# A three-stage kernel (WKV scan, MLP, routed experts) on one core: first expert's identity products, split order and one first level rearranged

## What is computed

```python
for t in range(S):                       # attention: B=2, H=8, S=768, D=48
    y[:, :, t] = r[t] . (state + (u*k[t]) outer v[t])
    state = w[t] * state + k[t] outer v[t]
x = relu(y @ w_in) ** 2 @ w_out          # MLP: 384 -> 2048 -> 384
expert = argmax(x @ w_gate)              # 8 experts, capacity 384 tokens each
out[i] = gate[i] * (relu(x[i] @ w1[expert]) @ w2[expert])   # 384 -> 1024 -> 384
```

## Time and profile before

| | |
|---|---|
| median of 3 runs | 496.4 us (495.31 to 496.63) |
| the profiled execution | 497.71 us |
| its span (first to last instruction) | 496.0 us |
| mean granted TensorE clock | 0.975 of full speed |
| TensorE busy | 457.9 us (92%) |
| VectorE busy | 317.0 us (64%) |
| ScalarE busy | 212.4 us (43%) |
| GpSimd busy | 53.6 us (11%) |

### The profile page before, as it was taken

How to read it: one execution, slowest core, us unless ns; L and a number is a source line. 1 busy time by engine, 2 the same in 40 slices (tenths; PEclk the granted TensorE clock), 3 DMA queues, 4 the chain that set the end, 5 groups by cost and what they waited for, 6 DMA issues and landing times.

```text
span 496.0 us, 15154 instructions
## 1 busy us (share of the span) xinstructions
PE 457.9 (92%) x6363; PEld 433.3 (87%) x6363; DVE 317.0 (64%) x805; ACT 212.4 (43%) x429; POOL 53.6 (11%) x64
## 2 busy tenths in 40 slices
PE   3678999999999999999999999998899988999993
PEld 3568989999999999999999899988899778989993
DVE  4985986777577756775677644435563778687510
ACT  2342463243523342434243444353365876676320
POOL 5000000000100010001000100101002334232301
PEclk9985999999999999999999999998899999999998
DMA  8941585680050005000000149201928798620000
GB/s 268 340 146 50 200 281 184 216 307 3 35 177 3 3 35 177 2 3 35 3 3 1 35 156 354 81 1 59 313 64 284 216 370 278 218 59 7 29 14 27
DMA packets 35356, 62.45 MB, mean 126 GB/s; under 512 B 3564, under 2 KB 21918, under 8 KB 35280
## 3 DMA queue, kind: packets, MB, share of 16 engines
q1 hardware_dynamic: 32976, 56.89, 33.9%
q0 software_dynamic: 2304, 4.47, 2.4%
HBM read 49.78 MB, written 14.19 MB: 129 GB/s over the span
## 4 chain that ended last, share of the span: by engine, by line
PE 70%; DVE 15%; issue 7%; ACT 4%; DMA 1%; SPq 0%; DVEq 0%; POOL 0%; ACTq 0%; POOLq 0%
PE bank L635 18%; PE bank L621 16%; PE bank L809 5%; PE pair L546 4%; PE pair L503 4%; PE bank L762 3%; PE pair L777 3%; PE bank L816 3%; PE bank L777 2%; DVE W L1021 2%; DVE KRW L1050 2%; DVE AD L1062 2%; PE pair L762 2%; DVE KRW L1049 2%; PE pair L567 2%
## 5 line engine op out<-in xcount | busy, mean ns | idle before, releaser
L621 PE MATMUL bank<-XH,W 128*128 128x256 f32 x576 | 121.9, 288 | 0.0
L635 PE MATMUL bank<-W,GH 128*128 128x384 f32 x384 | 102.3, 347 | 0.7 <-ACT X L848 0.7
L621 PEld LDWEIGHTS bank<-XH,W 128*128 128x128 f32 x576 | 96.3, 191 | 1.5 <-ACT RB L927 0.8
L848 ACT ACTIVATE GH<-GG 128x256 fp32r<-128x256 f32 x96 | 40.2, 419 | 115.6 <-DVE GG L1106 114.9
L621 PE MATMUL bank<-XL,W 128*128 128x256 f32 x288 | 81.5, 283 | 0.0
L1110 DVE TENSOR_TENSOR GL<-GG,GH 128x256 fp32r<-128x256 f32 x96 | 40.6, 423 | 41.9 <-ACT GH L848 41.9
L635 PEld LDWEIGHTS bank<-W,GH 128*128 128x128 f32 x384 | 64.1, 188 | 2.1 <-DVE GL L1110 1.0
L635 PE MATMUL bank<-W,GL 128*128 128x384 f32 x192 | 64.7, 337 | 0.0
L546 PE MATMUL pair<-KRW 48*64 48x32 f32 (+1 forms) x2304 | 48.1, 231 | 15.6 <-DMA KRW<-in_krw 6.4
L546 PEld LDWEIGHTS pair<-KRW 48*64 48x64 f32 (+1 forms) x2304 | 42.3, 146 | 22.9 <-issue 11.5
L927 ACT ACTIVATE RB<-bank 128x256 f32<-128x256 f32 x96 | 36.4, 379 | 44.4 <-PE bank L621 44.0
(11 more groups left out here) (139 smaller groups left out, 718.7 us busy)
## 6 DMA issues: line engine op xcount, KB each, us to landing
raw<-in_moe_w SPq DMA_DIRECT2D x23, 768.0 KB, 7.8
stage<-in_moe_w SPq DMA_DIRECT2D x9, 768.0 KB, 7.3
KRW<-in_krw SPq DMA_DIRECT2D x12, 512.0 KB, 6.1
slots<-X SPq DMA_DIRECT2D x8, 579.0 KB, 4.8
VV<-in_v SPq DMA_DIRECT2D x12, 288.0 KB, 9.2
XG<-slots SPq DMA_DIRECT2D x16, 193.0 KB, 3.1
KRW<-in_krw SPq DMA_DIRECT2D x12, 256.0 KB, 6.3
stage<-in_moe_w_in SPq DMA_DIRECT2D x4, 768.0 KB, 6.7
```

What stands on the lines that cost most here:

```text
L621: last = nc.tensor.matmul(bank[4 + f % 2][:, 0:2 * P], win[wa][:, c, f * P:(f + 1) * P], xa[:, c, :], start=n == 0, stop=n == 3 * KM - 1)
L635: last = nc.tensor.matmul(bank[6 + m][:, 0:DM], ga[f % G4][:, cols], wout[wa][:, f, :], start=f == 0 and n == 0, stop=f == NF - 1 and n == 2)
L848: return nc.scalar.activation(dst, src, ACT.Copy)
```

## The change

The slots of the first low splits become 5, 6, 7. On TensorE, level 0 and diagonal of group 1's tile 1 go behind `hidden(0, 0)`. The first expert's rows get banks `XB0` = 2, 3, 4; the identity products of tiles 0 and 1 are issued right behind the logits of the last group, ahead of its ranks; that of tile 2 stays where it was, and the wait for `rank_used` is gone. ScalarE and VectorE take all three tiles of expert 0's rows before the splits of chunks 2 and 3. VectorE's `gates` of expert 0 go behind its last `hidden_low` (or ahead of `hidden_low_small`, if that runs alone). The split of the last chunk of experts 4, 6 and 7 goes from behind f = 2 to behind f = 4, on both engines.

```diff
@@ -41,7 +41,7 @@
     KEYS = (10, 13)
     ZS, ZO = 8, 4
     HIGH_SLOT = (0, 1, 2, 3, 17, 19, 21, 23)
-    LOW_SLOT = (6, 7, 8, 18, 20, 22, 26, 29)
+    LOW_SLOT = (5, 6, 7, 18, 20, 22, 26, 29)
     ROWS, LOGITS, CHOOSE, RANKS, PLACE = range(5)
     GATE_SLOT = (4, 6, 7, 8, 9)
     PL = 3
@@ -135,6 +135,7 @@
         SB = (5, 2)
         SMALL = {0: (2, 4), 2: (7, 3)}
         XB = (0, 1, 4)
+        XB0 = (2, 3, 4)
         pair = [ctx.enter_context(nc.psum_tensor(f"pair{t}", [P, 2, 512], F32)) for t in range(2)]
         bank = [pair[n // 2][:, n % 2, :] for n in range(4)]
         bank += [ctx.enter_context(nc.psum_tensor(f"bank{n}", [P, 512], F32)) for n in range(4, 8)]
@@ -661,12 +662,18 @@
                                         start=False, stop=True)
                 last.then_inc(rank_done, 1)
 
+            def first_rows_early(m):
+
+                for q in range(KM):
+                    nc.tensor.matmul(bank[XB0[m]][:, q * P:(q + 1) * P], early[m][:, q * P:(q + 1) * P], ident[:, :],
+                                     start=q == 0, stop=False, skip_group_check=True)
+
             def attention(i, s, late):
 
                 n, k = due(i, s)
                 if n is None or late != (k == 0 or k > NL + 1):
                     return
-                for t in range(2):
+                for t in range(1 if (n, k) == (1, 0) else 2):
                     if k < NL:
                         level(n, t, k)
                     if k == 0:
@@ -684,6 +691,9 @@
                 for s in range(NF):
                     if mlp:
                         hidden(i - 1, s)
+                    if (i, s) == (1, 0):
+                        level(1, 1, 0)
+                        diagonal(1, 1)
                     if attn:
                         attention(i, s, False)
                     if mlp:
@@ -701,6 +711,11 @@
                         if attn:
                             pe.wait_ge(sel[0], NMASK * i + 4)
                         logits(i - 2)
+                        if i == NG + 1:
+                            pe.wait_ge(ld_early, 16 * MT)
+                            pe.wait_ge(relu_ready, NF * NG)
+                            for m in range(2):
+                                first_rows_early(m)
                     if RANKS in parts:
                         if attn:
                             pe.wait_ge(sel[0], NMASK * i + 5)
@@ -719,26 +734,16 @@
                 need(pe, xl2_ready, MT * e)
                 transposes(bank[XB[m]], XG[m], KM, xt2_done)
 
-            def first_rows_early(m):
-
-                for q in range(KM):
-                    nc.tensor.matmul(bank[XB[m]][:, q * P:(q + 1) * P], early[m][:, q * P:(q + 1) * P], ident[:, :],
-                                     start=q == 0, stop=False, skip_group_check=True)
-
             def first_rows_late(m):
 
                 for q in range(KM):
                     for n in range(2):
-                        last = nc.tensor.matmul(bank[XB[m]][:, q * P:(q + 1) * P], X2[:, n, q * P:(q + 1) * P],
+                        last = nc.tensor.matmul(bank[XB0[m]][:, q * P:(q + 1) * P], X2[:, n, q * P:(q + 1) * P],
                                                 chosen[n][:, m * P:(m + 1) * P], start=False, stop=n == 1,
                                                 skip_group_check=True)
                 last.then_inc(xt2_done, 1)
 
-            pe.wait_ge(ld_early, 16 * MT)
-            pe.wait_ge(rank_used, NG)
-            pe.wait_ge(relu_ready, NF * NG)
-            for m in range(MT):
-                first_rows_early(m)
+            first_rows_early(2)
             pe.wait_ge(slot_ready, NG)
             nc.tensor.matmul(bank[6][:, 0:NE], ones[:, :], earlier[:, 0, :], start=True, stop=True).then_inc(count_done, 1)
             pe.wait_ge(chosen_ready, 1)
@@ -944,12 +949,11 @@
             def rows_high(e, m):
                 act.wait_ge(xt2_done, MT * e + m + 1)
                 copy(XH2[:, :, m * P:(m + 1) * P],
-                     bank[XB[m]][:, 0:DM].rearrange("p (c n) -> p c n", c=KM)).then_inc(xh2_ready, 1)
-
-            for m in range(2):
+                     bank[(XB if e else XB0)[m]][:, 0:DM].rearrange("p (c n) -> p c n", c=KM)).then_inc(xh2_ready, 1)
+
+            for m in range(MT):
                 rows_high(0, m)
             split_high_expert(0, 2)
-            rows_high(0, 2)
             split_high_expert(0, 3)
 
             def hidden_high(e):
@@ -957,7 +961,7 @@
 
                     act.wait_ge(h2_done, NFE * e + f + 1)
                     nc.scalar.activation(HH[:, f, 0:2 * P], bank[HB[f % 3]][:, 0:2 * P], ACT.Relu).then_inc(hh_ready, 1)
-                    if f == 2 and e > 0:
+                    if f == 4 and e > 0:
                         split_high_expert(e, CH - 1)
 
             def hidden_high_small(e, m, done, ready):
@@ -1255,7 +1259,7 @@
 
             def rows_low(e, m):
                 dve.wait_ge(xh2_ready, MT * e + m + 1)
-                tt(XL2[:, :, m * P:(m + 1) * P], bank[XB[m]][:, 0:DM].rearrange("p (c n) -> p c n", c=KM),
+                tt(XL2[:, :, m * P:(m + 1) * P], bank[(XB if e else XB0)[m]][:, 0:DM].rearrange("p (c n) -> p c n", c=KM),
                    XH2[:, :, m * P:(m + 1) * P].bitcast(F32), ALU.subtract).then_inc(xl2_ready, 1)
 
             def gates(e, m):
@@ -1272,13 +1276,14 @@
             nc.vector.tensor_copy(count_u[:, :], bank[6][:, 0:NE]).then_inc(counted, 1)
             dve.wait_ge(counted, 1)
             split_low_expert(0, 1)
-            for m in range(2):
+            for m in range(MT):
                 rows_low(0, m)
             split_low_expert(0, 2)
-            rows_low(0, 2)
             split_low_expert(0, 3)
-            for m in range(MT):
-                gates(0, m)
+
+            def first_gates():
+                for m in range(MT):
+                    gates(0, m)
 
             def hidden_low(e):
                 for f in range(NFE):
@@ -1286,11 +1291,15 @@
                     nc.vector.scalar_tensor_tensor(out=HL[:, f, 0:2 * P], in0=bank[HB[f % 3]][:, 0:2 * P], scalar=0.0,
                                                    in1=HH[:, f, 0:2 * P].bitcast(F32), op0=ALU.max,
                                                    op1=ALU.subtract).then_inc(hl_ready, 1)
-                    if f == 2 and e > 0:
+                    if f == 4 and e > 0:
                         split_low_expert(e, CH - 1)
+                if e == 0:
+                    first_gates()
 
             def hidden_low_small(e, m, high, ready):
-                if m == 0 and e > 0:
+                if m == 0 and e == 0:
+                    first_gates()
+                elif m == 0:
                     split_low_expert(e, CH - 1)
                 for c in range(2):
                     dve.wait_ge(high, NFE * e + (c + 1) * NFE // 2)
```

## The result

Median 491.01 us (489.23 to 492.71, six runs) against 496.51 (495.31 to 496.72, six runs): ratio 0.9893, interval 0.9866 to 0.9921, so 5.5 us or 1.1% faster.

A forecast was written before the change was run, and what follows sets the result against it. TensorE hardly rests from 48 to 331 us, so time is winnable only at start, passage and experts: 2.8 + 1.5 + 1.5 = 5.8 us off the profiled 497.71 gives 491.9, median 1.3 lower, 490.6; range 488.6 to 494.0.

The forecast's parts named there:

- Slots, 0.64: Start: low slots 5, 6, 7 bring TensorE's first level to 36.1 instead of 36.74, or gain nothing.
- Level behind `hidden(0,0)`, 2.15: Start: tile 1's level behind hidden(0,0) helps VectorE's level 1 start at 44.85 instead of 47.64; whole start 2.8 us.
- I take it to be back by 45: Start: TensorE's clock, at 0.50, returns by 45 us; before, it was back between 46 and 48.
- The stall's reading: Start: TensorE's 1.77 us stall is instructions behind the third stage tile's chunk load; expected gone or passed during hidden(0,0).
- stall or low clock stays, 1.0 instead of 2.8: Rival at the start: the stall or low clock stays, so 1.0 us is won and time is 492.4; chance 0.17.
- Identity products, 2.2: Passage to the experts: moving them between logits and ranks starts the late products at 339.6 instead of 341.83, 2.2 us.
- with the gap filled the clock should stay up: Passage: TensorE's clock, 0.50 during the old identity products, stays up once they fill its idle gap.
- Rows before the splits, 0.7 of it let go: Passage: expert 0's fourth slice comes at 349.5 instead of 351.04, so 1.5 of the 2.2 us stay.
- I expect the same fall of the clock afterwards: Behind the passage: one gap of some 2.5 us before the fourth slice, then the same clock fall as before.
- Gates, 0: Expert 0: late gates delay loading expert 1's rows to 360.8, wanted at 361.05; costs nothing, 0.2 us to spare.
- The rival of late rows: Rival: expert 1's rows land after 5.8 us, TensorE stalls 2.5 us, time 493.1; chance 0.10.
- Last split, 1.5: Later experts: split behind f = 4 removes waits of 0.67 and 0.80 us; gain 1.5, bounds 0.8 and 1.6.

The follow-up runs named there:

- e11: Changed kernel with expert 0's split of chunk 3 behind its fifth hidden part; ratio 0.9856 to the kernel before, median 488.91 us.
- e4: Kernel before in its own order, with the weight load of the third stage tile held back until the first hidden slices are done; ratio 0.9979 to the kernel before.
- e8: Changed kernel with expert 0's gates still later, behind the first low part of its third tile; ratio 0.9992 to the kernel before.
- e12: Changed kernel with expert 0's split of chunk 2 behind its fifth and of chunk 3 behind its last hidden part; ratio 0.9966 to the kernel before.
- e7: Kernel before with only the last chunk's split moved behind f = 4; ratio 0.9951 to the kernel before.
- e6: Kernel before with only the new row order (all three row tiles before the splits) and the late gates; ratio 1.0016 to the kernel before.
- e10: Changed kernel with the old row order (tile 2's rows after the split of chunk 2); ratio 0.9866 to the kernel before, median 488.96 us.
- e9: Changed kernel with expert 0's gates back in front of its hidden parts; ratio 0.9907 to the kernel before, median 490.27 us.
- e1: Kernel before with only the low slots 5, 6, 7; ratio 0.9978 to the kernel before.
- e3: Kernel before with both edits of the start (low slots, and tile 1's level and diagonal behind hidden(0,0)); ratio 0.9961 to the kernel before.
- e5: Kernel before with only the identity products of tiles 0 and 1 moved behind the logits, in banks 2 and 3; ratio 0.9978 to the kernel before.
- e2: Kernel before with only first level and diagonal of tile 1 behind hidden(0,0); ratio 0.9958 to the kernel before.

## Why the prediction was right, and where not

**Direction and size.** 490.6 was forecast, 491.01 measured, within the range; the span fell by 5.1 us where the sum was 5.8. The sum hides errors of both signs.

**Slots, 0.64.** The state chain starts at 31.47 (forecast 31.4), and the idle 1.00 us ahead of the low half says that ScalarE's high half is last, as forecast. But first level starts at 36.84, not 36.1. The step that failed is what releases TensorE's L603. The prediction weighed the last state instruction against an earlier one. It isn't the last, which ends at 33.93 in the changed kernel, behind L603's start at 33.64. But the earlier one, for which the code waits, was done at 32.47 in the kernel before and 33.14 in the changed one, and L603's wait ended at 33.27 and 33.53. That is 1.58 and 1.40 us behind the end of an instruction transfer (31.68 and 32.13): this is TensorE's entry 1217, and in all fourteen profiles it comes 1.4 to 1.6 us behind such an end. So a VectorE that is earlier or later by half a microsecond hardly moves it in these profiles. In the changed kernel L603 also takes 1.10 us at the low clock instead of 0.68, and the run is 0.26 us late already at its split (26.46). Counted from the split, level(1,0,0) comes after 10.38 us instead of 10.54: the stated bound "nothing" was nearly it. Over all profiles it comes after 9.87 to 10.65 us with the old slots (six, median 10.40) and 9.27 to 10.41 with the new ones (eight, median 10.10): 0.3 us, within what one code varies.

**Level behind `hidden(0,0)`, 2.15.** The mechanism held: from first level to VectorE's level 1 it takes 9.41 us instead of 10.90, so 1.5. The missing 0.65 is the step "I take it to be back by 45": the clock came back at 50. Where it was back at 40.8 (e11), level 1 stands at

```profile
44.61 0.74 DVE L1065 COPY_PREDICATED AD<-mask,pair 128x256 f32<-128x256 uint32 x1
```

8.08 us behind its first level, below the 8.75 of the forecast. The stall's reading (instructions behind the chunk's load) was right in the instructions and only in part in the load: e4 keeps 1.21 us of pause with the load gone, behind an instruction transfer like the others. That it would be "passed while `hidden(0,0)` runs" is what happened. The Trainium skill (Runtime: NRT & Kernel Launch, Instruction fetch mechanics), against which the prediction weighed it, says that fetching sequential instructions is mostly hidden. The trace agrees for most of the way: of the 38 places at multiples of 256 entries from 705 to 10178, TensorE stands at five in the kernel before. But the stall is one of these five, so that it would have another cause didn't come out. The rival (stall or low clock stays, 1.0 instead of 2.8) came half true: the stall went, the low clock stayed, and the start gave 1.4 at level 1 and 2.4 in all with the later pause of 0.57, which is not the change's: a pause of 0.57 to 0.93 us at that place (entry 2754) stands in seven of the fourteen profiles, with old and new code. To this extent the closeness of the total is luck.

**Identity products, 2.2.** Late products lead by 3.96 - 2.38 = 1.6. The failed step is "with the gap filled the clock should stay up": it fell at 333.3, so twelve products took 2.1 us, not 1.7, the ranks came 0.4 us late instead of 0.1, VectorE stood idle 0.83 us until they came, and the third tile's six took 1.51. Where it stayed up (e11) the late products start at 335.90, 5.79 before those of the kernel before, with a lead of 3.57 at the logits: 2.2, the forecast.

**Rows before the splits, 0.7 of it let go.** From the first late product to the fourth slice the prediction had 9.9 us and it took 10.03, so the step was right. What the text didn't ask is where the 0.7 went: it is the price of the new row order (0.88) less the gates (0.22). The first slices read tiles 0 and 1 alone, so tile 2's rows ahead of the splits only delay them. Net of the start's lead the passage gave 0.9 instead of 1.5, and the missing 0.6 is the late products' start (1.6 instead of 2.2), that is the clock.

**The clock behind the passage.** "I expect the same fall of the clock afterwards" was wrong: none came, worth 1.5 us (3.3 to 4.8 in the lead). And one came at 398 that nobody asked for, at 2.1 us. Neither is in the sum; together they nearly cancel, which is luck.

**Gates, 0.** Right, and near in its margin: "0.2 us to spare" against 1.0 measured, 0.7 of which is the landing (2.4 us for 3.1). The rival of late rows didn't occur in the changed kernel (landing 2.4 us), but is what stopped e8, e11 and e12.

**Last split, 1.5.** Too small: 1.0 + 0.3 + 1.0 = 2.3 in the changed kernel, 2.2 in e7. Its bound of 1.6 took each wait at the idle time in the brackets (0.67 and 0.80), and that is less than the wait costs: products follow one another every 0.12 us though each lasts 0.28, so an idle 0.80 at expert 7 puts the product 1.08 us behind the one before it (467.10 to 468.18), where without the wait it is 0.12 (463.05 to 463.17 in the changed kernel). The lead grows by 0.97 at this one product. Expert 6 gained 0.3 that the text gave nothing. The rival (a new wait before the outputs) didn't occur. Of the signs named, "waits only once, 0.7 us" didn't hold: besides expert 6 (0.52) there is a wait of 0.89 at expert 4's fourth slice, which isn't in the earlier trace rows; e6, with the early split, has 0.66 at the same slice, e7 0.23, so it isn't the split's.

**What stays open:** why some of the places at multiples of 256 entries stop TensorE and most don't, and what decides from run to run where the low clock begins and how long it lasts. The combination that e10 and e11 point to (old row order, split of chunk 3 late, gates in front of that split) wasn't tried.

## What to carry to other kernels

Move work that waits for nothing into an engine's idle gap, and then check whose wait is next: here each step gained in the passage is worth only what expert 1's gather, 1.0 us behind, allows. When reordering two engines' chores ahead of a consumer, ask which of the inputs its first instructions read; the rest can come later. Price a wait of TensorE by the distance between the starts of two products, not by the idle time in the brackets. And state a term that rests on the clock with both of its values, since below 1% the clock's stretches decide as much as the edits.

## What the runs showed of the hardware

TensorE's granted clock falls at about the same places in every profile, but not for the same time, and not in every run. At the start it is at 0.50 for 6.8 us (e8, e9, e11), 10.2 (e1, e3, e6), 13.7 (before, e4, e5, e7, e10) or 17.1 (changed, e2, e12); around 398 us it falls in seven of the fourteen profiles, in old and new code. The six runs of the changed kernel go from 489.23 us at a mean clock of 0.990 to 492.71 at 0.972, though not in step with it (490.17 at 0.976, 491.86 at 0.981), so differences below about 2 us between two single profiles say nothing unless the shift is read between two instructions.

TensorE stops in straight code at fixed counts of its entries, 256 or a multiple of it apart, 1.2 to 1.6 us behind the end of a 16384-byte transfer on the instruction queue. Behind 23 or 24 small products at the start this cost 0.95 to 1.77 us in all six profiles of the old order, and nothing in the eight of the new one, where nine wide products (2.2 us) stand ahead. At entry 10178 it cost 0.65 to 0.96 us in all fourteen.
